# Attention tiles of 512, 512 and four of 496 tokens in place of five of 512 and one of 448

## The reference

```python
# attention: u, v are (2, 3008, 256), z is (2, 3008, 64)
scores = (1 / S) * np.matmul(z, z.transpose(0, 2, 1))
attn = np.maximum(scores, 0.0) ** 2
x = u * np.matmul(attn, v)
# first feed-forward layer, d_ff 2048
h = x @ w_in
x = (h - np.tanh(h)) @ w_out
# second feed-forward layer, d_ff 1536
out = (sigmoid(x @ w_gate) * (x @ w_val)) @ w_out
```

## Time and profile before

| | |
|---|---|
| time, median of 3 runs | 1497.74 us (1497.09 to 1497.86) |
| span of the profiled execution | 1496.5 us |
| PE busy | 1491.7 us (100% of the span) |
| DVE busy | 1135.7 us (76%) |
| ACT busy | 949.3 us (63%) |
| attention, from the start to about | 480 us |

### The profile page before, as it was taken

The page is one execution under the profiler, slowest core; times in us unless marked ns, Lnnn a source line. Parts: engine busy times, 40 slices in busy tenths (PEclk is TensorE's granted clock), DMA queues, the critical chain, the costliest instruction groups (busy, mean ns, idle before and its releaser), DMA issues.

```text
span 1496.5 us, 21893 instructions
## 1 busy us (share of the span) xinstructions
PE 1491.7 (100%) x8796; PEld 1257.0 (84%) x8796; DVE 1135.7 (76%) x1417; ACT 949.3 (63%) x1284; POOL 0.5 (0%) x5
## 2 busy tenths in 40 slices
PE   9999999999999999999999999999999999999999
PEld 8888888888888888888888889888888888888898
DVE  8999989999987787777686777666666676666656
ACT  8677767777766666666666666655556555555654
POOL 0000000000000000000000000000000000000000
PEclk9999999999999999999999999999999999999999
DMA  4344422254434345453535446453636454544352
GB/s 141 138 162 154 151 80 89 89 210 159 159 121 171 116 153 187 155 196 131 211 140 184 155 171 236 176 190 127 246 127 217 156 200 172 191 179 190 134 211 88
DMA packets 36341, 241.79 MB, mean 162 GB/s; under 512 B 3600, under 2 KB 6672, under 8 KB 22928
## 3 DMA queue, kind: packets, MB, share of 16 engines
q1 hardware_dynamic: 36096, 240.17, 43.8%
q10 hardware_dynamic: 144, 0.23, 0.0%
HBM read 196.21 MB, written 44.17 MB: 161 GB/s over the span
## 4 chain that ended last, share of the span: by engine, by line
PE 100%; ACT 0%; issue 0%; DVE 0%
PE acc L551 25%; PE hidden L618 13%; PE hidden L623 13%; PE hidden L620 13%; PE acc L511 10%; PE acc L513 10%; PE acc L512 10%; PE hidden L538 6%; PE acc L717 0%; PE acc L731 0%; PE acc L724 0%; ACT part_hi L923 0%; ACT h L920 0%; ACT x_out L1021 0%; DVE part_lo L1149 0%
## 5 line engine op out<-in xcount | busy, mean ns | idle before, releaser
L1030 DVE TENSOR_TENSOR part_lo<-h,part_hi 128x1024 fp32r<-128x1024 f32 (+3 forms) x317 | 375.1, 1183 | 81.8 <-ACT part_hi L870 50.0
L862 ACT ACTIVATE snap<-hidden 128x512 f32<-128x512 f32 (+1 forms) x360 | 211.8, 588 | 250.5 <-PE hidden L623 250.1
L618 PE MATMUL hidden<-region 128*128 128x512 f32 (+1 forms) x840 | 324.0, 386 | 0.0
L620 PE MATMUL hidden<-region 128*128 128x512 f32 (+1 forms) x840 | 323.7, 385 | 0.0
L623 PE MATMUL hidden<-region 128*128 128x512 f32 (+1 forms) x840 | 323.5, 385 | 0.0
L551 PE MATMUL acc<-part_hi,region 64*128 64x512 f32 (+1 forms) x2256 | 286.2, 383 | 0.4 <-ACT part_hi L923 0.4
L1120 DVE TENSOR_TENSOR h<-hidden,snap 128x512 f32<-128x512 f32 (+1 forms) x252 | 170.6, 677 | 143.8 <-ACT snap L862 117.8
L511 PE MATMUL acc<-part_hi,region 128*128 128x512 f32 (+1 forms) x664 | 256.2, 386 | 0.0
L512 PE MATMUL acc<-part_lo,region 128*128 128x512 f32 (+1 forms) x664 | 256.1, 386 | 0.0
L513 PE MATMUL acc<-part_hi,region 128*128 128x512 f32 (+1 forms) x664 | 256.0, 386 | 0.0
L551 PEld LDWEIGHTS acc<-part_hi,region 64*128 64x128 f32 x2256 | 216.5, 184 | 38.6 <-issue 0.8
(11 more groups left out here) (69 smaller groups left out, 1150.5 us busy)
## 6 DMA issues: line engine op xcount, KB each, us to landing
region<-ready SPq DMA_DIRECT2D x33, 2304.0 KB, 8.7
region<-ready SPq DMA_DIRECT2D x51, 1408.0 KB, 5.9
ready<-region SPq DMA_DIRECT2D x6, 2304.0 KB, 7.4
ready<-region SPq DMA_DIRECT2D x8, 1408.0 KB, 5.8
xs<-x_out SPq DMA_DIRECT2D x20, 512.0 KB, 6.1
x_in<-xs SPq DMA_DIRECT2D x20, 512.0 KB, 7.8
snap<-vP SPq DMA_DIRECT2D x24, 256.0 KB, 2.6
u_in<-uT SPq DMA_DIRECT2D x10, 512.0 KB, 5.3
```

The costliest lines, as they stand in the source:

```text
L618: pe.matmul(dst, weights[0], x[0], start=i < 3, stop=False, skip_group_check=True)
L620: pe.matmul(dst, weights[0], x[1], start=False, stop=False, skip_group_check=True)
L862: act.activation(snap[:, g % 2, i, 0:w], hidden[:, CHAIN[g % 2], 0:w], ACT.Copy).then_inc(s_snap, 1)
L1030: return ve.tensor_tensor(dst, whole, hi.bitcast(F32), ALU.subtract)
```

## The change

The widths of a batch's six tiles become a table: 512, 512, 496, 496, 496, 496. The sum is 3008 as before. Starts of tiles follow from it: 0, 512, 1024, 1520, 2016 and 2512 in place of 0, 512, 1024, 1536, 2048 and 2560.

```diff
+TILE_WIDTHS = (512, 512, 496, 496, 496, 496)
+assert len(TILE_WIDTHS) == TPB and sum(TILE_WIDTHS) == SEQ and max(TILE_WIDTHS) <= TOK
+
+
 def tile_width(T):
-    return min(TOK, SEQ - T % TPB * TOK)
+    return TILE_WIDTHS[T % TPB]
+
+
+def tile_start(T):
+    return sum(TILE_WIDTHS[:T % TPB])
 
 
 def tile_token(T):
-    return T // TPB * SEQ + T % TPB * TOK
+    return T // TPB * SEQ + tile_start(T)
...
         def tile_columns(T):
-            return slice(T % TPB * TOK, T % TPB * TOK + tile_width(T))
+            return slice(tile_start(T), tile_start(T) + tile_width(T))
```

## The result

The changed kernel takes 1499.92 us (median of 21 runs, 1499.51 to 1500.38), the kernel before 1497.74 us beside it. The ratio is 1.0015, 95% interval 1.0009 to 1.0021: slower by 2.2 us, where 2.4 us less was forecast. In the profiled executions the span grows from 1496.5 to 1498.3 us. In brackets stands the 95% interval. e3, e4, e5 and e9 were executed once and are read by their traces.

The account below looks back on a forecast made before the run. PE's matmul slots were taken to bound the kernel, with no wait inside the attention. The slot term of -2.36 us, all others at nothing, took 1497.74 us to 1495.4 us; range 1493.8 to 1501.0 us.

Parts of the forecast that it names:

- 0.5 us of cover: Attention tile starts: DVE's low part ends near 0.49 us before PE reads it at 496 columns, so PE waits for nothing.
- The term itself: Attention matmul slots of both batches: 354 x (880.0 - 886.7) ns, a change of -2.36 us.
- s: Length of an attention matmul slot at 496 columns, forecast as 220.0 ns; 221.7 ns would mean no change.
- 31 pieces plus 2: The 496-column slot in units of 6.67 ns, the stream time of 16 columns: 31 for streaming, 2 as surplus.
- the likeliest case: All 496-column attention slots at 220.0 ns, 1495.4 us, own range 1493.9 to 1497.1 us; chance 0.60.
- a fraction: Rival: 496-column slots settle on no whole number of pieces, 222.7 or 224.4 ns, 1499.2 or 1501.6 us; chance 0.11.
- its first price, 1499.2 us: Fraction rival with 496-column slots at a surplus of 16.0 ns, s = 222.7 ns, +1.4 us.
- The floor from the weight load: At 448 columns a 184 to 188 ns weight load under the preceding matmul was taken not to fit a 200.0 ns slot.
- a surplus of 20.0 ns: Slot time beyond streaming at 448 columns, 206.7 against 186.7 ns; at 512 columns it is 13.3 ns.
- The two levels of the earlier trace at 448: Feed-forward slots of 448 columns take 206.7 ns in the first layer and 202.7 ns in the second.
- The open term: First feed-forward layer's last pair: its 360 slots of 448 columns might fall to 202.7 ns, -1.4 us; chance 1 in 10.
- The rule of the Trainium skill: Warm matmul slot of N / 2.4 + 2.5 ns, a straight line in width, so the change would sum to zero.

Follow-up runs that it names:

- e3: Kernel before, with the attention scores' start shifted by 0 to 256 columns, a shift set for each tile; span 1499.2 us.
- e4: Kernel before at old starts, with a matmul width of its own for each tile, 512 down to 432 columns, on PE alone; span 1482.2 us.
- e5: Changed kernel with scores at the old, aligned starts, but tile 3 shifted by 16 columns and tile 9 by 48; span 1497.9 us.
- e9: e5 with one step's 15 slots in tiles 4 and 10 made 512 columns wide on PE; span 1496.1 us.
- e1: Changed kernel, but the scores read from the old starts, multiples of 512, at the new widths; 1496.0 us, ratio to before 0.9988.
- e6: Changed kernel's widths with each token once and all starts on multiples of 512, 48 tokens moved into padding; 1496.04 us, ratio 0.9991 to before.
- e2: Kernel before, old widths 512 and 448, with the scores read from the new starts; 1498.69 us, ratio 1.0007.
- e11: e6 plus the feed-forward widths of e7, with twelve 512-column matmuls in each feed-forward pair's third unit; 1494.38 us, ratio 0.9986 to the kernel before.
- e10: Changed kernel with widths 512, 512, 512, 512, 496, 464, so only tile 5's start is misaligned; 1495.7 us, ratio 0.9995 to the kernel before.
- e7: Kernel before with feed-forward pairs at widths 512, 512 and four of 496, attention as before; 1502.04 us, ratio 1.0032.

## Why the prediction was wrong

**What held.** That only slots count, that no engine or transfer makes PE wait, and that DVE keeps near 0.5 us of cover at the tile starts. The term itself held where its condition did: 220.0 ns in tiles 2 and 8 after (but for their last steps), in all 496-column tiles of e1 and e6, and 2.2 us of span against the 2.36 forecast (e1).

**The step that failed** is the one that made s a function of the width alone: "That gives s = 206.7 + 13.3 = 220.0 ns, or 31 pieces plus 2". It was applied to all four tiles of a batch. The diff moves three tiles' starts off their multiples of 512 columns, and the working priced no start at all. In the kernel before every start is such a multiple, so no row of it could show what another one costs. e1 and e2 show it, and e3 gives the grain, 64 columns. The loss has two parts: the misaligned scores themselves, 1.1 us, and the larger one, 2.8 us, in attends whose own operands are aligned. The measured time is inside the range of 1493.8 to 1501.0 us, but above the 1497.1 us at which the likeliest case ends, and the change has the other sign.

**The outcome is the rival called a fraction** (chance 0.11), with 223.2 to 224.0 ns in three tiles of four. Its reading, that 496 may settle on no whole number of pieces, is what the trace shows in those tiles, and its steps of 3.34 to 3.37 us are the ones seen. That its first price, 1499.2 us, is so near to the measured 1499.92 us is in part luck: it had all four tiles at 222.7 ns, and the trace has one at 220 and three at 223 to 224, for a reason, the starts, that this rival didn't have either. The argument against it, that 512 never does so in the long stretches, was right about 512 and said nothing of 496: 512 comes back into step by itself, as tiles 6 and 7 of e5 and the wide step of e9 show, and 496 did so in one place of e11 alone.

**The floor from the weight load was wrong.** It was to explain why 448 carries a surplus of 20.0 ns. At 432 columns the slot is 195.9 ns in e4, below any such floor. Why 448 columns in step carry three pieces and not two stays open. The two levels of the earlier trace rows at 448 were the sign of the real thing: a stream in step at 206.7 ns or out of step at 202.7. I took them for a soft edge of the floor. For 448 the disturbed pace happens to be the faster, and for 496 the slower.

**The open term** (the first layer's last pair at the other level, -1.4 us, 1 in 10) is real, and e10 has it, untouched by its edit, as 1.3 us. In the changed kernel it stayed as before.

**The rule of the Trainium skill** (TensorE: Matmul & The Clock Gate, Back-to-back issue gap), N / 2.4 + 2.5 ns, gives 209.2 ns for 496 columns, against 220.0 and 223.3 here. Its result for the change, none, was nearer to the measured +2.2 us than my -2.4 us by accident: it knows neither the gain of 2.2 us of span that e1 shows nor the loss of 4.0 us by the starts.

**What stays open.** Why a stream has two paces and what sets them isn't shown, nor why 512 recovers and why 496 did once. What throws the feed-forward layers' stream out of step was argued for the first `acc` matmul of a pair only, and has no explanation for the `hidden` matmuls of the second layer.

## What to carry to other kernels

When tile widths change, list what else follows from them: the start of every slice that a matmul streams. Keep these on multiples of 64 fp32 columns, or put the odd one last, behind which nothing of the same width comes (e10; its slots show the gain, its time doesn't tell it from no change). When PE is the bound, read the distance between matmul starts tile by tile and not only the waits: here two stretches of equal shapes, with the same waits, differ by 1.5% a slot. If a stream settles on the slower pace, a dozen matmuls at the full 512 columns brought it back here for less than it lost (e11).

## What the runs showed of the hardware

All of it is for float32r operands at the 2.4 GHz clock (granted clock 1.00), with a weight load for each matmul.

- The steadiest slots (before, e1, e4, e6) are 226.7 ns at 512 columns, 220.0 at 496 and 488, 213.3 at 472 and 206.7 at 448: multiples of the 6.67 ns in which 16 columns stream.
- Widths 496 and 448 have a second pace, 223.3 and 202.7 ns. 496 kept it for 309 us (e7), 448 for over 60 us (the second feed-forward layer in every trace with such a pair). At 220.0 ns every slot is 220 ns long, while at 223.3 ns single slots vary from 221 to 227 ns (e11, 729 to 736 us). 512 was back at 226.7 ns after some eight slots (e9: eight slots at 231 ns in the mean), or 13 behind the starts of the shifts 4 and 16 (e3).
- A moving operand that starts off a multiple of 64 fp32 columns (256 bytes from the tensor's start) costs 3 to 7 ns a slot at 512 columns (e3), and disturbs the slots behind it, whose operands are aligned. A shift of 32 columns, 128 bytes, is not enough.
